# The eighth expert pair joins rows of upper and lower parts into one product, and four weight splits move behind its last quarter

## The reference

```python
# 1: linear attention with decay, state 64 x 64 for each of 4 x 8 heads, 768 steps
state = gamma * state + k_t v_t^T ;  y_t = scale * q_t state
# 2: a dense layer, 512 -> 2048 -> 512
h = x @ w_in ; g = max(h, 0) + alpha * min(h, 0) ; x = g @ w_out
# 3: each token goes to one of 8 experts, 512 -> 1024 -> 512
logits = normed(x) @ normed(expert_emb).T / tau ; e = argmax(logits)
out = softmax(logits)[e] * (max(x @ w1[e], 0) @ w2[e])
```

## Time and profile before

| | |
|---|---|
| median of 3 runs | 948.07 us (947.96 to 949.17) |
| the profiled execution | 947.68 us, span 945.6 us |
| PE busy | 934.3 us (99% of the span) |
| PE weight loads | 788.1 us (83%) |
| DVE busy | 667.5 us (71%) |
| ACT busy | 314.9 us (33%) |
| POOL busy | 261.1 us (28%) |
| HBM read and written | 124.16 MB and 26.31 MB |

### The profile page before, as it was taken

One profiled execution on the slowest core, in us unless ns is written; L12 is line 12 of the kernel. 1 busy time (PEld: TensorE's weight loads), 2 busy tenths in 40 slices (PEclk: granted clock), 3 DMA queues, 4 the chain that ended last, 5 costly groups with the idle time before them and its releaser, 6 DMA issues.

```text
span 945.6 us, 15972 instructions
## 1 busy us (share of the span) xinstructions
PE 934.3 (99%) x5537; PEld 788.1 (83%) x5537; DVE 667.5 (71%) x1180; ACT 314.9 (33%) x436; POOL 261.1 (28%) x193
## 2 busy tenths in 40 slices
PE   8999999999999999999999999999999999999996
PEld 7888888888888888888888888889988889888885
DVE  4555579747984698558965897786786667799641
ACT  4232121112111121112111221245566666678541
POOL 4443215331434134422433232512021111100101
PEclk9999999999999999999999999999999999999998
DMA  8432297024001500140002302168856668799611
GB/s 291 161 131 79 82 386 258 1 90 146 0 0 45 189 0 0 39 149 24 1 8 94 123 1 90 46 231 308 302 200 243 227 230 299 288 358 380 226 43 55
DMA packets 32898, 137.64 MB, mean 146 GB/s; under 512 B 5280, under 2 KB 5792, under 8 KB 24114
## 3 DMA queue, kind: packets, MB, share of 16 engines
q1 hardware_dynamic: 25186, 118.27, 34.8%
q0 software_dynamic: 4480, 12.74, 3.5%
q10 hardware_dynamic: 3168, 5.79, 1.8%
HBM read 124.16 MB, written 26.31 MB: 159 GB/s over the span
## 4 chain that ended last, share of the span: by engine, by line
PE 98%; DMA 1%; DVE 0%; SPq 0%; issue 0%; POOL 0%; POOLq 0%; ACT 0%
PE bank L796 28%; PE bank L814 28%; PE bank L958 16%; PE bank L889 6%; PE bank L927 5%; PE bank L922 3%; PE bank L682 2%; PE bank L726 2%; PE bank L698 2%; PE bank L781 1%; PE bank L924 1%; PE bank L715 1%; PE bank L937 1%; DMA attention<-in_qk 1%; PE bank L921 0%; DVE en_all L1058 0%
## 5 line engine op out<-in xcount | busy, mean ns | idle before, releaser
L796 PE MATMUL bank<-activations_split,weights_split 128*128 128x512 f32 x1152 | 277.7, 391 | 0.0
L814 PE MATMUL bank<-weights_split,activations_split 128*128 128x512 f32 x1152 | 276.3, 389 | 0.0
L814 PEld LDWEIGHTS bank<-weights_split,activations_split 128*128 128x128 f32 x1152 | 216.1, 188 | 45.2 <-POOL activations_split L1899 0.4
L796 PEld LDWEIGHTS bank<-activations_split,weights_split 128*128 128x128 f32 x1152 | 215.1, 188 | 45.9 <-issue 1.1
L1899 POOL TENSOR_TENSOR activations_split<-scratch,activations_split 128x512 fp32r<-128x512 f32 x84 | 123.6, 1472 | 301.8 <-ACT activations_split L1630 297.0
L1630 ACT CAST activations_split<-scratch 128x512 fp32r<-128x512 f32 x96 | 59.8, 622 | 409.8 <-DVE scratch L1101 409.8
L958 PE MATMUL bank<-weights_split,activations_split 128*128 128x512 f32 (+1 forms) x648 | 158.1, 395 | 0.0
L958 PEld LDWEIGHTS bank<-weights_split,activations_split 128*128 128x128 f32 x648 | 118.8, 188 | 23.3
L1096 DVE TENSOR_SCALAR scratch<-bank,alpha 128x512 f32<-128x512 f32 x96 | 71.7, 747 | 91.8 <-PE bank L796 90.8
L1329 DVE TENSOR_TENSOR weights_split<-attention,weights_split 128x2048 fp32r<-128x2048 f32 (+1 forms) x45 | 102.2, 2286 | 18.8 <-ACT weights_split L1710 18.6
L1958 POOL DMA_INDIRECT out<-scratch,y_token x27 | 38.6, 1429 | 261.3 <-ACT scratch L1743 260.7
(11 more groups left out here) (271 smaller groups left out, 865.7 us busy)
## 6 DMA issues: line engine op xcount, KB each, us to landing
attention<-in_w_exp SPq DMA_DIRECT2D x48, 1024.0 KB, 6.5
en_all<-in_w_exp SPq DMA_DIRECT2D x16, 1024.0 KB, 7.0
attention<-in_kv SPq DMA_DIRECT2D x43, 256.0 KB, 4.2
expert_rows<-in_pad_rows SPq DMA_DIRECT2D x8, 1285.0 KB, 25.4
rows<-in_w_mlp SPq DMA_DIRECT2D x14, 512.0 KB, 3.9
attention<-in_qk SPq DMA_DIRECT2D x12, 512.0 KB, 5.6
rows<-expert_rows ACTq DMA_DIRECT2D x22, 257.0 KB, 4.6
scratch<-in_qk SPq DMA_DIRECT2D x10, 512.0 KB, 3.6
```

What stands on the lines that cost most here:

```text
L796: last = mm(H_ps[f % 2][:, :], win(a, kc, f), x[:, kc, :], start=(k == 0), stop=(k == 3 * KC - 1))
L814: last = mm(bank[j][:, :], x[f % 2][:, j * P:(j + 1) * P], wout(a, f), start=(f == 0 and a == 0 and part_ == "hi"), stop=(f == FB - 1 and ...
```

## The change

WIDE now takes in pair 7, so that its first product is made as those of pairs 3 to 6 are, with the four steps behind each quarter. What stood between the quarters of pair 7 moves. The last chunk of set 7 is split where the wide pairs split theirs: on ACT behind the result of tile 13, on DVE behind the first sum. Set 8's chunks 0 and 1 are split behind the last quarter. Its chunks 2 and 3 are split behind the low and high parts of tile 16's rows. On ACT set 9's w1 moves behind the result of tile 15. The wait that protected the banks in the pair behind the last wide one goes, since no pair follows.

```diff
--- before.py
+++ after.py
@@ -316,7 +316,7 @@
     dot_out = [A[:, 9 * TB:10 * TB], bank[7][:, :]]
     EMB_ps = bank[7][:, 320:320 + KC * E].rearrange("p (k e) -> p k e", k=KC)
     TAU_ps = bank[7][:, 384:385]
-    WIDE = range(EARLY, PAIRS - 1)
+    WIDE = range(EARLY, PAIRS)
     EW_ps = [pair, lower]
 
     def sums(g):
@@ -903,9 +903,7 @@
                     else:
                         pe.wait_ge(s_lo[0], due(s_lo[0], HC * i))
                 used = 4 * (i - WIDE[0]) + g - 2
-                if i - 1 == WIDE[-1] and g < 2:
-                    pe.wait_ge(s_hs, due(s_hs, 4 * len(WIDE)))
-                elif i in WIDE and used >= 0:
+                if i in WIDE and used >= 0:
                     pe.wait_ge(s_hs, due(s_hs, used + 1))
                 elif i == WIDE[0] and g == 0:
                     pe.wait_ge(s_hl, due(s_hl, 4 * i))
@@ -1546,23 +1544,16 @@
             for i in range(3, PAIRS):
                 if i in WIDE and i > 3:
                     wide_groups(i)
-                if i == PAIRS - 1:
-                    h_two_low(i, 0)
-                    h_two_low(i, 1)
-                    split_expert(i, (3,))
-                    h_two_low(i, 2)
-                    split_expert(PAIRS, (0,))
-                    h_two_low(i, 3)
-                    split_expert(PAIRS, (1,))
                 if i + 1 < PAIRS:
                     split_expert(i + 1, (0,))
                     x_lo_part(2 * i + 2, 2 * i + 2)
                     split_expert(i + 1, (1,))
+                    x_lo_part(2 * i + 3, 2 * i + 3)
+                    split_expert(i + 1, (2,))
                 else:
+                    split_expert(PAIRS, (0, 1))
+                    x_lo_part(LEAD, LEAD)
                     split_expert(PAIRS, (2, 3))
-                x_lo_part(2 * i + 2 + (i + 1 < PAIRS), 2 * i + 2 + (i + 1 < PAIRS))
-                if i + 1 < PAIRS:
-                    split_expert(i + 1, (2,))
             w1_part(next_expert(LEAD))
             x_lo_part(LEAD + 1, 1)
             relu_half(LEAD)
@@ -1781,17 +1772,13 @@
                     if i not in WIDE:
                         split_expert(i, (3,))
                     h_two_high(i, 2)
-                    if not more:
-                        split_expert(PAIRS, (0,))
                     h_two_high(i, 3)
-                    if not more:
-                        split_expert(PAIRS, (1,))
                 if more:
                     split_expert(i + 1, (0,))
                     x_hi_part(t + 2, t + 2)
                     split_expert(i + 1, (1,))
                 else:
-                    split_expert(PAIRS, (2, 3))
+                    split_expert(PAIRS, (0, 1))
                 y_part(t, t // 4, t % 4)
                 if i == 2:
                     act.wait_ge(s_late, due(s_late, 1))
@@ -1802,12 +1789,14 @@
                     load_rows(act, t // 4 + 1, t % 4)
                 x_hi_part(t + 2 + more, t + 2 + more)
                 if not more:
-                    w1_part(next_expert(LEAD), LEAD - 1)
+                    split_expert(PAIRS, (2, 3))
                 elif i + 1 >= EARLY:
                     split_expert(i + 1, (2,))
                 y_part(t + 1, t // 4, t % 4 + 1)
                 if i + 1 in WIDE:
                     split_expert(i + 1, (3,))
+                if not more:
+                    w1_part(next_expert(LEAD), LEAD - 1)
                 if 2 <= i and more:
                     load_rows(act, t // 4 + 1, t % 4 + 1)
             relu_half(LEAD)
```

## The result

| | before | changed |
|---|---|---|
| median | 948.07 us | 954.44 us |
| runs | 947.96 to 949.17 | 953.02 to 954.55 |
| span of the profiled execution | 945.6 us | 952.4 us |
| mean granted clock of PE | 0.997 | 0.994 |

The medians differ by 6.4 us. The ratio, which is an estimate of its own and not the quotient of the medians, is 1.0061, with a 95% interval of 1.0044 to 1.0079, so the change costs between 4.2 and 7.5 us. The time lies in the stated range (950.8 to 954.6), but it is not my likeliest case, 952.0: it is rival B, forecast at 954.0.

What follows compares the result with a forecast made beforehand. Bound by what PE issues plus waits, near the edit by how late tile 17's low part stands in DVE's queue. The profiled 947.68 us plus a 4.16 us stall gave 951.84, by the median 952.23, stated as 952.0; range 950.8 to 954.6.

Steps and rivals of the forecast that it cites:

- likeliest case: Tile 17's up product on PE: the stall alone, 952.0 us, bounds 951 to 953.2; chance 0.55.
- rival B: Behind the stall at tile 17: PE's clock also falls to half, 1.4 to 2.75 us more, 954.0; chance 0.25.
- (1): Pair 7's first product on PE: 64 matmuls instead of 96, a gain of 0.21 us.
- (2): Four steps instead of two behind each quarter of pair 7, on ACT and DVE: hidden, cost nothing.
- (3): Set 7's last chunk on DVE: subtracted 4 us earlier, nobody waits for it, cost nothing.
- (4): Set 8's late chunks delay set 9's w1 and tile 17's low part: PE's weight load 4.16 us later.
- (5): Behind the stall: PE stays busy, so the delay remains; bunched loads cost nothing, otherwise up to 2 us.
- main case: The same as the likeliest case: tile 17's stall alone, 952.0 us, range 951.0 to 953.2; chance 0.55.
- Rival C: Set 9's or set 10's first chunks land late and ACT waits: 1 to 2 us more, 953.5; chance 0.07.
- D: Tile 17's weight load: not slower, set 8's late chunks cost ACT and DVE nothing before 804, 947.9 us; chance 0.12.
- neutral outcome: Whole kernel: no change that a measurement can tell, within about 0.2% (1.9 us); chance 0.12.

Runs made afterwards that it cites:

- e3: Changed kernel with pair 7 (the eighth) narrow again and the splits left where the change put them: 954.34 us, ratio 1.0079.
- e1: Changed kernel with casts and subtractions of set 8's chunks 2 and 3 cut to 16 of 2048 columns: 953.38 us, ratio 1.0064.
- e5: As e1, and the loads of set 9's w1 chunks 0 and 1 fetch only 16 columns: 951.76 us, ratio 1.0045.
- e6: As e5, with set 9's w1 on ACT ahead of tile 15's result again: 949.08 us, ratio 1.0019.
- e4: Changed kernel, set 8's splits between and behind pair 7's quarters, set 9's w1 ahead of tile 15's result, as before the change: 951.93 us, ratio 1.0045.
- e8: Against e4, set 8's chunk 0 is subtracted between the second quarter's sum and low part, chunk 1 behind the last low part: 949.78 us, ratio 1.0020.
- e9: Against e8, ACT casts set 8's chunk 1 between the third quarter's copy and rectification: 948.42 us, ratio 1.0010.
- e10: The changed kernel unaltered, run again on one chip with a filler kernel: 954.27 us, ratio 1.0067.
- e7: Changed kernel with 18 filler matmuls of 128 columns, whose result nobody reads, on PE in the pause ahead of tile 17: 953.22 us, ratio 1.0054.

## Why the prediction was right, and where it was not

**(1) The pair's shape: right.** From the row of tile 13's last twelve matmuls to tile 14's first it was 791.11 - 776.74 = 14.37 us, and is 791.09 - 776.94 = 14.15: 0.22 us, forecast 0.21.

**(2), (3) The four steps and set 7's chunk: right.** Tile 14's products follow without a wait (8.33 us for 36, before 8.35).

**(4) The stall: right in place and size, with one link left out.** PE's first weight load of tile 17 starts at 812.46, forecast 812.72. The delay is 3.90 us, where 4.16 stood in the sum. The sum ran through ACT's queue: set 8's two late casts, tile 15's result, set 9's first cast, and DVE 0.35 us behind it. The trace has that chain, each step within 0.3 us. What the sum left out is the load of set 9's second chunk. It looked at the first chunk alone, and only as a bound that needs the longest landing. The second, issued at 799.79 and landed 7.15 us later, bound just as much: the queue alone makes 3.89 us (e3), the load alone makes 3.89 us (e1), and w1 behind tile 15's result comes third (e5, e6). The number came out since the two chains tie. Whoever had followed the sum and taken set 8's late casts and subtractions out of the way would have gained nothing on the stall, as e1 shows.

**(5) Behind the stall: right within 0.22 us** for the changed kernel, which I had put at nothing. It is more when PE comes to the loads sooner, as in the kernels with fillers and, less, in e1 and e3.

**The clock: the mis-sized term.** The main sum had it at nothing and gave it a chance of 0.25 as rival B, at 1.4 to 2.75 us. The clock fell in each profile with a pause of 3.9 to 4.2 us (the changed kernel twice, e1, e3) and in none where the longest was 2.76 us or less (e4, e5, e6, e8, e9). That is no safe line between them: in e10 it fell 2.1 us after PE's last matmul, in e1 3.8 us. What I had in hand already said so: at the end of the program the clock falls some 3 us after the last matmul, and the forecast pause was 4.6 us. That the pause was longer than the one case on record should have made B the likeliest, at 952.0 + 2.1, and not the "luckier pause" my text asks for. The decomposition of the 6.8 us by which the span grew: the stall 3.90, the half clock 2.62 (6.52 us behind at 818.71, less 3.90), late loads 0.22; together 6.74.

The Trainium skill (TensorE: Matmul & The Clock Gate, "HAM oscillation") says that a wait between bursts brings the throttle back and costs half the throttled time. The trace agrees, with 5.48 us for a row of 2.75.

One sign of the prediction's main case failed with it: every later row of PE was to be as long as before and 4.2 us later. The first is 5.48 us long and the rest stand 6.5 to 6.7 us later. The range holds 954.44 only because it took in most of B; by the main case alone, 951.0 to 953.2, it would have been missed.

Rival C, late loads on top of the stall, had a small part: ACT waited 0.49 us for set 9's second chunk, which the queue nearly hid, and late loads cost 0.22 us behind it, not 1 to 2. D and the neutral outcome had none. D asked that set 8's late chunks cost nothing: e1 made them cost nothing and the stall stayed. Two readings in the prediction were wrong without a part in the sum. DVE was not idle for 0.7 us ahead of 800.56 but for 0.1 (it ended at 798.16 + 2.29 = 800.45), and that end of its last subtraction lies behind the transposes of tile 16's rows at 799.30 and not ahead of them.

## What to carry to other kernels

Before moving work past a point in a queue, follow all that hangs on it: here the same move lengthened the queue ahead of set 9 and delayed set 8's first subtractions, and with them the issue of set 9's loads (the second went out at 799.79, before at 796.23), so that removing either cost alone leaves the stall as it is. A few cheap cuts, singly and together, show this sooner than a sum along one chain. And where TensorE will stand for longer than any pause in the trace, look at what its clock did behind the longest one that is there, and price the stall with the slow stretch behind it: two tenths of a microsecond of better shape were bought with six.

## What I had not expected of the hardware

- The slow stretch is not of one length. In the changed kernel the granted clock was 0.50 from about 811.3 to 818.0, and in e1 only from about 811.4 to 814.8, with PE busy from 811.5; tile 17's twelve matmuls took 5.48 and 4.54 us. The other two profiles fall in with these: 6.8 us of half clock in e10, 3.4 in e3. From tile 17's first matmul to its second half it was 6.24 us in the changed kernel, 5.82 in e10, 5.17 in e1 and 4.99 in e3, against 3.64 in e7 at full clock. So its cost on the spot differs by more than a microsecond between profiles, from 1.35 to 2.6 us. A single run of the changed kernel at 953.02 us with a mean clock of 0.997 stands beside three at 954.4 to 954.6 with 0.994.
- A slow stretch of PE can give time back. The half clock cost 2.6 us on the spot and some 1.2 to 1.6 in the end (the fillers' 0.9 us and their own 0.3, or 2.6 less 1.0), as late loads seem to be hidden by it. Both ends of this are estimates from the differences above.
- A plain fp32 matmul of 128 columns is recorded twice and takes 0.23 us (72 records in 8.20 us for 36 instructions), while the transposes of the same shape take 0.11 (four in 0.44 us on the chain of e5).
